# Last block of a two-layer gated MLP chain: the output product turned round, tokens on partitions, three copies and three stores in place of two transposes and four stores

## What is computed

```python
qn = q / (norm(q, over tokens) + 1e-6);  kn = k / (norm(k, over tokens) + 1e-6)
a = softmax(kn.T @ qn / tau)                  # 256 x 256, over the last axis
x = v @ a                                     # 6016 x 256
# layer 1
xn = x / sqrt(mean(x * x) + 1e-6) * rms_g
g = xn @ w1_gate
y = (silu(g) * (xn @ w1_val)) @ w1_out        # F = 1536 in between
# layer 2
gate = sigmoid(y @ w2_gate)
out = (gate * (y @ w2_val)) @ w2_out          # 6016 x 256
```

## Time and profile before

| | us |
|---|---|
| three runs | 1250.82, 1250.99, 1252.98 |
| median | 1250.99 |
| the profiled execution's own time | 1251.03 |
| its span in the profile | 1249.2 |
| around the span (1251.03 - 1249.2) | 1.83 |
| granted TensorE clock, mean | 0.999 of full |

### The profile page before, as it was taken

The page is one execution under the profiler, slowest core; times in us unless marked ns, Lnnn a source line. Parts: engine busy times, 40 slices in busy tenths (PEclk is TensorE's granted clock), DMA queues, the critical chain, the costliest instruction groups (busy, mean ns, idle before and its releaser), DMA issues.

```text
span 1249.2 us, 15542 instructions
## 1 busy us (share of the span) xinstructions
PE 1237.9 (99%) x5580; PEld 1039.9 (83%) x5580; DVE 685.6 (55%) x1140; ACT 456.4 (37%) x741; POOL 30.3 (2%) x25
## 2 busy tenths in 40 slices
PE   8999999999999999999999999999999999999998
PEld 7888888888888888888888888888888888889888
DVE  6787654655555555555455455555455555546343
ACT  5554533333333333333333333333333333333332
POOL 0001600000000000000000000000000000000000
PEclk9999999999999999999999999999999999999999
DMA  9930000100100100000010010010010000000000
GB/s 345 315 90 1 1 1 9 35 0 8 34 0 8 34 0 8 22 12 0 8 34 0 8 34 0 8 34 0 8 34 0 8 8 21 1 7 17 1 18 13
DMA packets 62322, 37.01 MB, mean 30 GB/s; under 512 B 51288, under 2 KB 54744, under 8 KB 62296
## 3 DMA queue, kind: packets, MB, share of 16 engines
q1 hardware_dynamic: 61496, 36.47, 10.2%
q10 hardware_dynamic: 800, 0.20, 0.1%
HBM read 30.48 MB, written 6.18 MB: 29 GB/s over the span
## 4 chain that ended last, share of the span: by engine, by line
PE 98%; DMA 1%; DVE 0%; ACT 0%; SPq 0%; issue 0%; DVEq 0%; ACTq 0%
PE ps L831 21%; PE ps L832 21%; PE ps L833 21%; PE ps L971 10%; PE ps L970 10%; PE ps L969 10%; PE ps L921 3%; DMA qk<-in_k 1%; PE ps L882 0%; SPq L285 0%; PE ps L875 0%; PE ps L904 0%; PE ps L863 0%; DVE out_sb L547 0%; PE ps L864 0%
## 5 line engine op out<-in xcount | busy, mean ns | idle before, releaser
L764 DVE TENSOR_TENSOR h<-ps,h 128x512 f32<-128x512 f32 (+1 forms) x276 | 187.7, 680 | 248.8 <-PE ps L833 236.6
L472 ACT ACTIVATE h_hi<-h 128x512 fp32r<-128x512 f32 (+1 forms) x276 | 171.6, 622 | 365.2 <-DVE h L764 363.6
L467 ACT ACTIVATE h<-ps 128x512 f32<-128x512 f32 (+1 forms) x276 | 162.2, 588 | 327.2 <-PE ps L833 315.5
L769 DVE TENSOR_TENSOR h_lo<-h,h_hi 128x512 fp32r<-128x512 f32 (+1 forms) x276 | 190.6, 691 | 139.1 <-ACT h_hi L472 137.2
L971 PE MATMUL ps<-h_hi,w_lo_o 128*128 128x512 f32 (+1 forms) x576 | 221.7, 385 | 0.0
L969 PE MATMUL ps<-h_hi,w_hi_o 128*128 128x512 f32 (+1 forms) x576 | 221.7, 385 | 0.0
L970 PE MATMUL ps<-h_lo,w_hi_o 128*128 128x512 f32 (+1 forms) x576 | 221.6, 385 | 0.0
L760 DVE TENSOR_TENSOR h<-ps,h 128x512 f32<-128x512 f32 (+1 forms) x132 | 89.7, 679 | 136.7 <-ACT h L467 136.7
L969 PEld LDWEIGHTS ps<-h_hi,w_hi_o 128*128 128x128 f32 x576 | 108.2, 188 | 20.7
L970 PEld LDWEIGHTS ps<-h_lo,w_hi_o 128*128 128x128 f32 x576 | 108.2, 188 | 20.5
L971 PEld LDWEIGHTS ps<-h_hi,w_lo_o 128*128 128x128 f32 x576 | 108.1, 188 | 20.5
(11 more groups left out here) (139 smaller groups left out, 1338.8 us busy)
## 6 DMA issues: line engine op xcount, KB each, us to landing
v_in<-in_v SPq DMA_DIRECT2D x44, 128.0 KB, 2.9
out<-out_sb SPq DMA_DIRECT2D x44, 128.0 KB, 2.4
qk<-in_q SPq DMA_DIRECT2D x10, 512.0 KB, 7.1
qk<-in_k SPq DMA_DIRECT2D x10, 512.0 KB, 9.3
w_raw_g<-in_moe_w_gate SPq DMA_DIRECT2D x6, 512.0 KB, 7.8
w_raw_v<-in_moe_w_val SPq DMA_DIRECT2D x6, 512.0 KB, 8.3
w_raw_o<-in_moe_w_out SPq DMA_DIRECT2D x6, 512.0 KB, 9.0
scratch<-root_row SPq DMA_DIRECT2D x9, 256.0 KB, 3.1
```

The source lines that it names most:

```text
L467: nc.scalar.activation(h[:, slot, 0:w], ps[:, GATE[slot], 0:w], ACT.Sigmoid).then_inc(sig_done, 1)
L472: nc.scalar.activation(h_hi[:, part, 0:w], h[:, slot, 0:w], ACT.Copy).then_inc(hi_done, 1)
L764: nc.vector.tensor_tensor(h[:, slot, 0:w], ps[:, VALUE[slot], 0:w], h[:, slot, 0:w], ALU.mult).then_inc(h_done, 1)
L769: nc.vector.tensor_tensor(h_lo[:, part, 0:w], h[:, slot, 0:w], h_hi[:, part, 0:w].bitcast(F32), ALU.subtract).then_inc(lo_done, 1)
```

## The change

Only the last block's layer-two output is touched. The gated values become the stationary operand (128 tokens of `h_hi` or `h_lo` at a time, `down_tokens`), and the 256 output channels of the output weights' row block are the moving columns. So a tile's `down` is three token groups i of 128 tokens, each three matmuls of 256 columns, into three banks (`LAST`), and the result lies with tokens on partitions and all 256 channels in a row. No turn is needed; three copies (`copy_last`: groups 0 and 2 on ScalarE, 1 on VectorE) put the banks into `out_sb`, laid out anew as `last_sb`, and put back the order of the channels: the output weights of layer two are kept with even channels ahead of odd ones, so the copy reads a bank as "(d m)" and writes "(m d)". Three stores of 128 pieces of 1 KB (`store_last`) follow: groups 0 and 1 from SP's queue, 2 from ScalarE's. The DRAM side of a store is walked as 4 x 32 x 256 elements (s, t, channel), the on-chip side is 128 partitions x 256. The last tile signals each group by itself (`last_part`), the others still signal `down_done` once per tile.

```diff
@@ -49,7 +49,7 @@
     TAIL = N - FULL * BLOCK
     BLOCKS = FULL + 1
     LAG = 2
-    assert CC == 2 and N % P == 0 and 0 < TAIL and FULL >= 4 and J % 6 == 0
+    assert TAIL // P == 3 and CC == 2 and N % P == 0 and 0 < TAIL and FULL >= 4 and J % 6 == 0
 
 
     sizes = [1, 2] + [QK_TILES] * ((TILES - 7) // QK_TILES) + [2, 2]
@@ -148,6 +148,8 @@
         GATE, VALUE = (0, 2), (1, 3)
         Y, X = (4, 5), (6, 7)
         RAW, NORM, SPREAD = (0, 1), (2, 3, 4, 5), 2
+        LAST = (Y[0], Y[1], X[0])
+        last_sb = out_sb[:, :, :].rearrange("p s m -> p (s m)").rearrange("p (i c) -> p i c", c=C)
 
         ssq = small[:, 0:4]
         norm = small[:, 4:8]
@@ -199,7 +201,8 @@
         hi_done, lo_done, down_done = sem("hi_done"), sem("lo_done"), sem("down_done")
         y1_copied, y2_turned = sem("y1_copied"), sem("y2_turned")
         x2_hi_done, x2_lo_done = sem("x2_hi_done"), sem("x2_lo_done")
-        out_free, last_half = sem("out_free"), sem("last_half")
+        out_free, last_part = sem("out_free"), sem("last_part")
+        last_copied = [sem(f"last_copied{i}") for i in range(TAIL // P)]
 
 
 
@@ -245,11 +248,18 @@
         block = ctx.enter_context(nc.Block())
 
 
-        def store_last(eng, quarters):
-
-            eng.wait_ge(y2_turned, BLOCKS * CC)
-            for quarter in quarters:
-                eng.dma_start(rows(out, FULL)[quarter], row_tile(out_sb, FULL, quarter)).then_inc(out_free, 16)
+        def copy_last(copy, wait, i):
+
+            wait(last_part, i + 1)
+            wait(out_free, BLOCKS * 16 * QUARTERS)
+            copy(last_sb[:, i, :].rearrange("p (m d) -> p d m", d=CC),
+                 ps[:, LAST[i], 0:C].rearrange("p (d m) -> p d m", d=CC)).then_inc(last_copied[i], 1)
+
+        def store_last(eng, i):
+
+            eng.wait_ge(last_copied[i], 1)
+            part = out[FULL * BLOCK:N, :].rearrange("(t s) c -> s t c", s=TAIL // SQ)[i * QUARTERS:(i + 1) * QUARTERS]
+            eng.dma_start(part, last_sb[:, i, :]).then_inc(out_free, 16)
 
         @block.sync
         def _(sp):
@@ -306,8 +316,9 @@
             spread_root(FULL)
             store_out(FULL - 2)
             store_out(FULL - 1)
-            store_last(sp, (0, 1))
-            sp.wait_ge(out_free, 16 * QUARTERS * (BLOCKS + 1))
+            store_last(sp, 0)
+            store_last(sp, 1)
+            sp.wait_ge(out_free, 16 * (QUARTERS * BLOCKS + TAIL // P))
 
 
         @block.gpsimd
@@ -517,7 +528,9 @@
                     layer(seq2(b), width(b), mid, end)
 
             plan(Walk())
-            store_last(act, (2, 3))
+            copy_last(nc.scalar.copy, act.wait_ge, 0)
+            copy_last(nc.scalar.copy, act.wait_ge, 2)
+            store_last(act, 2)
 
 
         @block.vector
@@ -538,9 +551,7 @@
             def turn_y2(b, c):
 
                 w = width(b)
-                if isinstance(b, int) and b == FULL:
-                    dve.wait_ge(last_half, c + 1)
-                elif c == 0:
+                if c == 0:
                     dve.wait_ge(down_done, seq2(b) * J + J)
                 if c == 0:
                     dve.wait_ge(out_free, b * 16 * QUARTERS + 16 * QUARTERS)
@@ -812,8 +823,7 @@
                     layer(seq2(b), width(b), None, extras,
                           {1: [(turn_y2, b - 1, c) for c in range(CC)]} if last else {})
                     if last:
-                        for c in range(CC):
-                            turn_y2(b, c)
+                        copy_last(nc.vector.tensor_copy, dve.wait_ge, 1)
 
             plan(Walk())
 
@@ -958,6 +968,14 @@
                         pe.wait_ge(y2_turned, b * CC)
                     else:
                         pe.wait_ge(y1_copied, (b + 2) * CC)
+                if layer == "2" and isinstance(b, int) and b == FULL:
+                    for i in range(TAIL // P):
+                        mm = down_tokens(j, i)
+                        if j == J - 1:
+                            mm.then_inc(last_part, 1)
+                    if j < J - 1:
+                        mm.then_inc(down_done, 1)
+                    return
                 for d in range(CC):
                     mm = down_half(layer, j, d, w)
                 mm.then_inc(down_done, 1)
@@ -970,11 +988,13 @@
                 nc.tensor.matmul(dst, hi, h_lo[:, part, 0:w], start=False, stop=False)
                 return nc.tensor.matmul(dst, lo, h_hi[:, part, 0:w], start=False, stop=(j == J - 1))
 
-            def last_down():
-
-                pe.wait_ge(lo_done, seq2(FULL) * J + J)
-                for d in range(CC):
-                    down_half("2", J - 1, d, TAIL).then_inc(last_half, 1)
+            def down_tokens(j, i):
+
+                dst, part = ps[:, LAST[i], 0:C], j % (LAG + 1)
+                h_i, l_i = (t[:, part, i * P:(i + 1) * P] for t in (h_hi, h_lo))
+                nc.tensor.matmul(dst, h_i, w_hi["o2"][:, j, :], start=(j == 0), stop=False)
+                nc.tensor.matmul(dst, h_i, w_lo["o2"][:, j, :], start=False, stop=False)
+                return nc.tensor.matmul(dst, l_i, w_hi["o2"][:, j, :], start=False, stop=(j == J - 1))
 
             class Walk:
                 eng = pe
@@ -1024,9 +1044,8 @@
                         if not last and not before_last:
                             self.next_x(j, b + 2, xs)
                     if last:
-                        for tile in self.due[:-1]:
+                        for tile in self.due:
                             down(*tile)
-                        last_down()
 
                 def next_x(self, j, b, vt):
                     if j == 0 and narrow(b):
```

## The result

The changed kernel takes 1252.89 us (median of 20 runs, 1252.36 to 1253.67), the kernel before 1250.97 beside it (20 runs, 1250.38 to 1252.98): ratio 1.0014, 95% interval 1.0008 to 1.0021. It is 1.9 us slower, less than the 0.2% within which the prediction calls it the same; 1252.7 was forecast.

What follows compares the result with a forecast made beforehand. TensorE, busy 99% of the span, and the end after its last matmul bound the kernel. Last matmul +0.42 us, then copies, issue and 4.2 us of four-engine flow end the span at 1250.9: +1.7 on 1251.03 gives 1252.7, range 1249.9 to 1254.2.

Steps and rivals of the forecast that it cites:

- Part 1: Last block's `down` tiles: nine 256-column matmuls at 0.120 us replace six of 384, +0.04 us a tile, +0.48 for twelve.
- The f32 row of 256 columns: Plain f32 matmul row, 0.215 us apart, taken as the upper end for the 256-column matmuls: +10.3 us.
- One bound: Floor for the last block's 108 matmuls if weight loads set 0.111 us: stated as -0.5 us against 0.120.
- the 0.120 case: Last block's 256-column matmuls taken as 0.120 us apart, from 0.1733 - 0.0533.
- Part 2: Last tile: the small stall of 0.06 us goes, just covered; the last matmul ends at 1244.93, 0.42 us later.
- Part 3: Three PSUM copies replacing turns: about 0.38, 0.42, 0.38 us, none waiting for another, the last done at 1245.36.
- Part 4: Store issue: 0.6 us on SP, 0.76 on ScalarE's queue; first issue 0.5 us earlier, last starts 0.5 us earlier.
- Part 5: Last stores: the same four DMA engines carry all three, 4.2 us of flow, span ends 1250.9, +1.7 us.
- the flow: Data movement of the three last stores: 98304 bytes an engine at 23.5 GB/s, 4.2 us, from 1245.9 to 1250.1.
- Sixteen engines: Rival at the last stores: all 16 DMA engines take part, time 1250.2, range 1250.0 to 1250.5; chance 0.23.
- The low rate: Rival at the last stores: four engines below 19.6 GB/s each, near 12.9 the end is 1256.1; chance 0.09.
- The distance of 256-column matmuls: Rival in all 12 `down` tiles: load or f32r form sets over 0.1275 us; at 0.215 time is 1263.0; chance 0.08.

Runs made afterwards that it cites:

- the run with one queue: Changed kernel with store 2 also issued from SP's queue, so all three stores come from one queue: 1252.76 us, ratio 1.0012 to the kernel before.
- 12 and 32: Kernel before with only its four last stores' DRAM side walked 12 x 32 x 64 instead of 32 x 12 x 64: 1255.26 us, ratio 1.0031.
- the 8 x 16 neighbouring rows: Changed kernel with last-block tokens in natural order, each store's DRAM side written as 8 x 16 rows at the same addresses: 1249.12 us, ratio 0.9985.
- the 16-count run: Changed kernel with last-block tokens in natural order, each store walking 16 x 8 rows, inner step 16 rows: 1250.12 us, ratio 0.9995 to the kernel before.
- the natural order: Changed kernel with last-block token s*32 + t in column s*32 + t, each store writing 128 successive DRAM rows: 1249.27 us, ratio 0.9986 to the kernel before.

## Why the prediction was right, step by step

**Part 1, the matmuls.** Right, a little high: 1.07 us for nine, 0.119 apart, for 0.120; over the block +0.34 where +0.42 was summed. The weight loads cost nothing over the straight line from 512 and 384 columns. Whether the 256 columns or the load set the 0.119 us isn't told apart, since loads by themselves came 0.111 to 0.122 us apart. The f32 row of 256 columns (0.215) was no guide for this form. One bound was misread: 0.111 us is 0.5 us under the kernel before, as 108 x 0.111 = 12.0 against 72 x 0.1733 = 12.5, but 1.0 us under the 0.120 case; the forecast doesn't use it.

**Part 2, the last tile.** Right: no wait is left in the stream; the last group runs at the distance of the others.

**Part 3, the copies.** 0.39, 0.42 and 0.38 us for 0.38, 0.42, 0.38, and none waits for another.

**Part 4, the issue.** SP 0.635 for 0.6. ScalarE's 1.39 for 0.76 is wrong, and the run with one queue shows that it is not on the path.

**Part 5, the engines.** Right, and it decides the sign: 4 completions a store, a share of a quarter, 95 GB/s where 94 was worked out. The rule of the Trainium skill ("DMA: Bandwidth & Descriptors", "Why a DMA increments its semaphore by 16 and not by 1"), the largest number up to 16 that divides both outermost counts, agrees with every run here: 4 and 128 gave 4, 12 and 32 gave 4, 8 and 16 gave 8 and 16 (8 only where the rows weren't neighbours; the 8 x 16 neighbouring rows gave 16). The 12 and 32 part it from the smaller of the two counts, which the prediction had taken. The term that was undersized is the flow, 4.7 us for 4.2: its first 0.9 us run at 20 to 64 GB/s. That span 1251.0 came out near the 1250.9 forecast is in part luck: the flow's 0.5 too much was met by the TensorE's 0.08 less and the 0.30 of earlier start in this execution. Measured inside the traces the loss is 0.34 + 1.8 = 2.1; the medians, 1252.89 - 1250.97 = 1.92, are 0.2 over the 1.7.

**The rivals.** Sixteen engines was priced at 1250.2 and the 16-count run shows 1250.12: the price was right and the condition not met. The low rate did not come: 1 KB pieces run at 23.8 GB/s an engine. The distance of 256-column matmuls stayed below 0.1275. The stated range, 1249.9 to 1254.2, would have held the sixteen-engine case too, so it is the traces, not the time alone, that decide for four engines.

So the change is made of a part that gains and a part that loses more. Turned output, copies and 1 KB pieces come to 1249.27 against 1251.05 beside it, when the stores use all engines and write neighbouring rows. With all engines but scattered rows they come to 1250.12 against 1251.16, a ratio of 0.9995 (0.9986 to 1.0004) that can't be told from no change. The walk of the stores as 4 x 32 rows costs 3.6 us against the natural order, 2.8 of it against sixteen engines with scattered rows.

## What to carry to other kernels

Before a store on the last path is reshaped, look at the outermost count of both its sides: in every run here the largest number up to 16 that divides both was how many DMA engines carried it, and the packets over the data packets in a trace say how many did. If a layout forces a small outer count, change the order in which the data is laid out at the input, where it cost nothing here (the load of v for the last block), rather than the walk of the store. Stores of neighbouring rows were a few tenths of a us quicker in issue and landing, which can count where a store is the last thing a kernel waits for.

## What the hardware showed that was not expected

- The issue of a 128 KB store took 0.42 us on SP and 0.37 on ScalarE's queue with neighbouring rows, 0.61 and 0.67 with scattered rows on 16 engines, and 1.50 and 1.39 on ScalarE's queue with 8 and 4 engines, behind SP's two.
- Four engines were each faster than sixteen: 18 GB/s against 12.9 with 256-byte pieces, 23.8 against 323 / 16 = 20.2 with 1 KB pieces.
- The changed kernel's stores on four engines begin at 20 to 31 GB/s for about half a microsecond, are at 87 from 1 us on and hold 95 later; with eight engines the flow was uneven and took 3.2 us (about 1245.6 to 1248.8) for the 2.05 worked out.
- A separate 128x128 load for each 256-column matmul added nothing to the stream over the straight line from the wider matmuls (0.119 us apart), though loads by themselves came 0.111 to 0.122 us apart; the two are too near to say which sets the distance.
